# Token tiles in blocks of 1, eight times 2, and 1, instead of nine times 2, with the expert weights split further ahead in the short blocks

## The reference, cut to what matters

```python
def _moe_ref(x, w_gate, w1, w2):          # first mixture: N, D, E, F = 2304, 512, 8, 1024
    P = ...                               # gates of each token and expert, 8 rounds of normalising
    for e in range(E):
        h = np.maximum(x @ w1[e], 0.0)
        out += P[:, e:e + 1] * (h @ w2[e])
    return out

def _moe2_ref(x, phi, w1, w2):            # second mixture: 32 slots
    logits = x @ phi
    d = softmax of logits over the tokens
    slot_input = (d.T @ x).reshape(E, S_per_e, D)
    for e in range(E):
        slot_out[e] = np.maximum(slot_input[e] @ w1[e], 0.0) @ w2[e]
    c = softmax of logits over the slots
    return c @ slot_out
```

## Time and profile before

| | us |
|---|---|
| median of three runs | 1754.67 (1753.51 to 1755.44) |
| the profiled execution | 1753.28 |
| its span, first to last instruction | 1751.5 |
| PE busy | 1700.8 (97%) |
| PE weight loads (beside PE) | 1305.2 |
| DVE busy | 1024.3 (58%) |
| ACT busy | 776.9 (44%) |
| POOL busy | 418.8 (24%) |
| granted clock of PE, mean | 0.988 |
| moved by DMA | 258.57 MB |

### The profile page before, as it was taken

One profiled execution on the slowest core, in us unless ns is written; L12 is line 12 of the kernel. 1 busy time (PEld: TensorE's weight loads), 2 busy tenths in 40 slices (PEclk: granted clock), 3 DMA queues, 4 the chain that ended last, 5 costly groups with the idle time before them and its releaser, 6 DMA issues.

```text
span 1751.5 us, 31771 instructions
## 1 busy us (share of the span) xinstructions
PE 1700.8 (97%) x13225; PEld 1305.2 (75%) x13225; DVE 1024.3 (58%) x1306; ACT 776.9 (44%) x1161; POOL 418.8 (24%) x319
## 2 busy tenths in 40 slices
PE   7999999999999999999999999999999999999975
PEld 6888888888876877777777777777777777777434
DVE  6888787878754555555555555555555555555201
ACT  3444444444466444444444444454444444444101
POOL 3788888888810000000000000000000000000000
PEclk9999999999999999999999999999999999999997
DMA  9531322322035444443443444444434434454998
GB/s 300 144 82 42 79 45 65 59 46 52 15 133 193 157 151 141 142 144 133 145 145 132 155 135 141 137 141 136 145 133 146 147 131 153 156 192 167 386 420 337
DMA packets 159390, 258.57 MB, mean 148 GB/s; under 512 B 46784, under 2 KB 65216, under 8 KB 153536
## 3 DMA queue, kind: packets, MB, share of 16 engines
q1 hardware_dynamic: 159248, 256.54, 44.7%
HBM read 251.79 MB, written 9.96 MB: 149 GB/s over the span
## 4 chain that ended last, share of the span: by engine, by line
PE 63%; DMA 3%; DVE 2%; ACT 2%; issue 1%; SPq 0%; DVEq 0%
PE ring L1062 44%; PE ring L1072 7%; PE ring L1084 4%; PE ring L1119 4%; DMA wring<-in_moe_w_dram 2%; DMA xraw<-in_moe_w_dram 1%; PE ring L974 1%; DVE w_lo L1350 1%; PE ring L985 1%; ACT w_hi L1248 1%; PE ring L1170 1%; PE ring L1190 1%; ACT x_split L1240 0%; PE ring L1095 0%; ACT hring L1255 0%
## 5 line engine op out<-in xcount | busy, mean ns | idle before, releaser
L1062 PE MATMUL ring<-w_hi,x_split 128*128 128x512 f32 x2304 | 790.8, 404 | 3.3 <-DVE w_lo L1350 2.5
L1062 PEld LDWEIGHTS ring<-w_hi,x_split 128*128 128x128 f32 x2304 | 432.8, 188 | 116.7 <-issue 24.6
L1062 PE MATMUL ring<-w_lo,x_split 128*128 128x512 f32 x1152 | 449.9, 391 | 0.0
L1350 DVE TENSOR_TENSOR w_lo<-w_raw,w_hi 128x1024 fp32r<-128x1024 f32 x288 | 356.6, 1239 | 155.5 <-ACT w_hi L1248 155.5
L1293 ACT ACTIVATE wring<-ring,pw 128x512 f32<-128x512 f32 x218 | 150.1, 689 | 435.5 <-PE ring L1062 435.5
L1392 DVE COPY h_t<-ring 128x512 f32<-128x512 f32 x288 | 199.1, 691 | 236.6 <-PE ring L1072 236.5
L584 POOL TENSOR_TENSOR acc<-acc,pt 128x576 f32<-128x576 f32 x210 | 297.5, 1417 | 28.1
L1248 ACT ACTIVATE w_hi<-w_raw 128x1024 fp32r<-128x1024 f32 x288 | 302.6, 1051 | 0.0
L1528 POOL TENSOR_TENSOR x_split<-xraw,x_split 128x512 fp32r<-128x512 f32 (+1 forms) x20 | 23.6, 1185 | 980.0 <-ACT x_split L1240 980.0
L515 DVE TENSOR_REDUCE neg_part<-ring 116x2 f32<-116x768 f32 (+1 forms) x240 | 228.8, 958 | 43.7 <-PE ring L303 24.4
L1062 PEld LDWEIGHTS ring<-w_lo,x_split 128*128 128x128 f32 x1152 | 217.5, 189 | 37.9
(11 more groups left out here) (212 smaller groups left out, 1692.8 us busy)
## 6 DMA issues: line engine op xcount, KB each, us to landing
w_raw<-in_moe_w_dram SPq DMA_DIRECT2D x288, 512.0 KB, 3.5
wring<-in_moe_w_dram SPq DMA_DIRECT2D x34, 1024.0 KB, 10.0
q_raw<-in_q_dram SPq DMA_DIRECT2D x32, 288.0 KB, 5.9
v_raw<-in_v_dram SPq DMA_DIRECT2D x16, 576.0 KB, 4.5
xraw<-in_moe_w_dram SPq DMA_DIRECT2D x9, 1024.0 KB, 14.7
k_raw<-in_k_dram SPq DMA_DIRECT2D x30, 288.0 KB, 7.1
hring<-in_moe_w_dram SPq DMA_DIRECT2D x6, 1024.0 KB, 21.1
out_dram<-wring SPq DMA_DIRECT2D x8, 512.0 KB, 6.1
```

What stands on the lines that cost most here:

```text
L1062: last = pe.matmul(h_ps[n % 3][:, :], a[:, k, toks], w[:, k, :], start=(k == 0 and m == 0), stop=(k == DK - 1 and m == 2))
L1350: dve.tensor_tensor(w1_lo[v % 2][:, 2 * c:2 * c + 2, :], w1_raw[:, 2 * (p % RAWS):2 * (p % RAWS) + 2, :], w1_hi[v % 2][:, 2 * c:2 * c + 2, ...
```

## The change

The blocks become 1, eight times 2, and 1 tile: 10 blocks instead of 9, so the first mixture's weights are read ten times. In a block of one tile a unit lasts one tile; there both of its pieces are split two units ahead, four pieces ahead of the first tile, and PE waits for them one at a time. The raw ring has 4 places, the ring of hidden tiles 36 slots instead of 38. `G_AT` becomes 4, 9, 17, 25 and for a block of one 4, 9, 11, 13. With a last block of 16 tiles, five ring places are read for the last time ahead of it, and both halves of the raw ring are places. x's two buffers go by the tile's parity instead of its place in the block; in a block's last unit ACT splits x and the weights ahead of its copy. The last group of transposes of w2 @ phi moves behind the first hidden tile, the one before it to the end of its loop.

```diff
-SPARE_UNITS = [6, 7, 8, 9, 10]
+SPARE_UNITS = [10, 11, 12, 13, 14]
-    BLOCKS = [2] * (TT // 2)
+    BLOCKS = [1] + [2] * (TT // 2 - 1) + [1]
-    RAWS = 3
+    RAWS = 4
-    SLOTS_H = 38
+    SLOTS_H = 36
-    G_AT = [5, 9, 17, 25]
+    G_AT = {1: [4, 9, 11, 13], 2: [4, 9, 17, 25]}
+    SPLIT_EARLY = 4
...
+    def last_of(t):
+
+        b = max(b for b in range(NB) if T0[b] <= t)
+        return N0[b] + BLOCKS[b] * (UNITS - 1) + t - T0[b]
+
+    def single(v):
+
+        return BLOCKS[v // UNITS] == 1
+
+    def pieces_up_to(n):
+
+        b, u, i = place_of(n)
+        v = global_unit(b, u)
+        if single(v) or (i == 1 and v + 1 < UNITS * NB and single(v + 1)):
+            ahead = PIECES * (v + 3)
+        else:
+            ahead = PIECES * (v + 2) + i
+        return min(ahead, PIECES * UNITS * NB)
+
+    def pieces_at(n):
+        before = max([SPLIT_EARLY] + [pieces_up_to(m) for m in range(max(0, n - 3), n)])
+        return range(before, max(before, pieces_up_to(n)))
...
         PLACES = [("x", behind_c(i), TT) for i in range(3)] \
             + [("slots", four(i), last_user(i)) for i in EARLY_RING] \
-            + [("slots and logits", (wring[:, 22:24, :], unit_rows(4)), last_user(22, 2))] \
-            + [("raw", w1_raw[:, 0:4, :], W1_PIECES - 1)] \
+            + [("raw", w1_raw[:, 4 * i:4 * i + 4, :], W1_PIECES - 2 + 2 * i) for i in range(2)] \
...
-            EARLY_AT = [PIECES * UNITS * (NB - 1) + n for n in (6, 10, 14)]
+            EARLY_AT = [PIECES * UNITS * (NB - 1) + n for n in (4, 10, 16)]
...
-                if i % 16 == 8 and i > 16:
+                if i % 16 == 8 and 16 < i < STEPS - 16 + 8:
                     turn_phi(i // 16 - 1)
+            turn_phi(QUADS - 2)
             times_phi(QUADS - 1, (0, 1, 2, 3))
-            turn_phi(QUADS - 1)
...
                 if i == 0:
-                    pe.wait_ge(w_low, PIECES * (v + 1))
+                    pe.wait_ge(w_low, PIECES * v + 1 if single(v) else PIECES * (v + 1))
...
                 for k in range(DK):
+                    if single(v) and k == DK // PIECES:
+                        pe.wait_ge(w_low, PIECES * (v + 1))
...
                 hidden(n)
+                if n == 0:
+                    turn_phi(QUADS - 1)
...
-                if i in (18, 22, 34):
-                    split_w1((18, 22, 34).index(i))
+                if i in (18, 22, 34, 50):
+                    split_w1((18, 22, 34, 50).index(i))
...
+                urgent = u == UNITS - 1 and i == 0 and BLOCKS[b] == 2
+                if urgent:
+                    split_x(T0[b] + 2)
+                    for p in pieces_at(n):
+                        split_w1(p)
                 keep(n)
-                if u == UNITS - 1 and b + 1 < NB:
-                    split_x(b + 1, i)
+                if u == UNITS - 1 and not urgent and T0[b] + i + 2 < TT:
+                    split_x(T0[b] + i + 2)
...
-                if i == 0 and v + 1 < UNITS * NB:
-                    split_w1(PIECES * (v + 1) + 1)
-                if i == BLOCKS[b] - 1 and v + 2 < UNITS * NB:
-                    split_w1(PIECES * (v + 2))
+                for p in pieces_at(n) if not urgent else ():
+                    split_w1(p)
```

More of the change, by code:

```diff
@@ L668, in quad_before, with tokens_at @@
         return QUADS * b + u // COLS + 1
+    def last_of(t):
[14 more added lines that the diff above has]
+        return range(before, max(before, pieces_up_to(n)))
+    def tokens_at(t):
+        return slice(t % 2 * P, (t % 2 + 1) * P)
     ctx = ExitStack()
@@ L815, in last_user @@
             return max(QUADS * place_of(n)[0] + place_of(n)[1] // COLS + 1 for n in tiles)
-        RING_PLACES = sorted([i for i in range(0, 4 * (SLOTS_H // 4), 4) if i != 20], key=last_user)
+        RING_PLACES = sorted([i for i in range(0, 4 * (SLOTS_H // 4), 4) ], key=last_user)
         EARLY_RING = [i for i in RING_PLACES if last_user(i) <= G_ALL - QUADS]
         LATE_RING = [i for i in RING_PLACES if last_user(i) > G_ALL - QUADS]
-        g_rows = [wring[:, 20, :], wring[:, 21, :], w1_raw[:, 4, :], w1_raw[:, 5, :]]
+        G_PLACE = LATE_RING.pop()
+        g_rows = [four(G_PLACE)[:, q, :] for q in range(QUADS)]
         W1_PIECES = PIECES * UNITS * NB
@@ L862, in tail @@
             i = place_of_load[k]
[L863 removed]
+            return PLACES[i][1], tail_in[i], 16 * load_count[k]
         def first_load(e, n):
@@ L942, in load_tail @@
                     sp.dma_start(place_halves(place)[1], rows[:, FB // 2:FB, :]).then_inc(last_in, 16)
-                elif isinstance(place, tuple):
-                    for half, part in enumerate(place):
-                        sp.dma_start(part, rows[:, 2 * half:2 * half + 2, :]).then_inc(arrived, 16)
                 else:
@@ L1234, in _, with split_x @@
         def _(act):
[L1235 to L1240, removed]
+            def split_x(t):
+                if t >= 2:
+                    act.wait_ge(h_made, last_of(t - 2) + 1)
+                for batch, s, rows, o in tokens_of(t * P, P):
+                    last = act.activation(x_hi[:, :, tokens_at(t)][:, :, o:o + rows], xraw[:, batch * DK:(batch + 1) * DK, s:s + rows], ACT.Copy)
                 last.then_inc(x_high, 1)
@@ L1270, in _ @@
                 if i == EARLY_QUADS:
-                    for x in range(BLOCKS[0]):
-                        split_x(0, x)
-                if i in (18, 22, 34):
-                    split_w1((18, 22, 34).index(i))
+                    for x in range(2):
+                        split_x(x)
+                if i in (18, 22, 34, 50):
+                    split_w1((18, 22, 34, 50).index(i))
                 if i == 15:
@@ L1279, in _ @@
                     keep_wp(i // 16 - 1)
-                if i % 16 == 8 and i > 16:
+                if i % 16 == 8 and 16 < i < DK * UNITS - 16 + 8:
                     keep_phi(i // 16 - 1)
+            keep_phi(QUADS - 2)
             keep_wp(QUADS - 1)
@@ L1382, in _ @@
                 dve.tensor_tensor(pw[:, :, :], pw[:, :, :], col[:, :].unsqueeze(1).broadcast_to([P, TT, E]), ALU.mult).then_inc(scaled, 1)
-            for p in range(PIECES + 1):
+            for p in range(SPLIT_EARLY):
                 split_w1(p)
@@ L1473, in _ @@
                         keep_c(b - 1)
[L1474 to L1479, removed]
+                    if at in G_AT[BLOCKS[b]]:
+                        add_g(b - 1, G_AT[BLOCKS[b]].index(at), g_ps)
+                for p in pieces_at(n):
+                    split_w1(p)
             keep_turned(TILES - 1)
@@ L1522, in _ @@
             pool.memset(ones[:, :], 1.0).then_inc(ones_set, 1)
[L1523 to L1529, removed]
+            for t in range(TT):
+                pool.wait_ge(x_high, t + 1)
+                for batch, s, rows, o in tokens_of(t * P, P):
+                    at = slice(t % 2 * P + o, t % 2 * P + o + rows)
+                    last = pool.tensor_tensor(x_lo[:, :, at], xraw[:, batch * DK:(batch + 1) * DK, s:s + rows], x_hi[:, :, at].bitcast(F32), ALU.subtract)
+                last.then_inc(x_low, 1)
             pool.wait_ge(z_made, QUADS * NB)
```

24 lines of the change are left out of this document (10 added, 14 removed).

## The result

The changed kernel takes **1769.5 us** (median of six runs, 1766.9 to 1771.0) against 1755.1 before, a ratio of 1.0078 with a 95% interval from 1.0059 to 1.0098: slower by 14.5 us, where 5.9 had been forecast. The sign was right, the size was not, and the time lies outside the range of 1753 to 1768. The profiled execution took 1768.52 with a span of 1766.7, 15.2 more than before.

What follows compares the result with a forecast made beforehand. PE bounds the kernel up to the last expert tile, then the remaining weights' transfer. PE's +6.0 and waits of +1.5 put the last hidden product at 1636.3; weights end +5.9 later, giving 1760.6 us, range 1753 to 1768.

Steps and rivals of the forecast that it cites:

- The bounds and the sign: Whole kernel: PE bounds up to the last expert tile, then the remaining weights' transfer; slower by 5.9 us.
- rival 2: Tail: last piece still goes out 16.6 us ahead, so the gain pays for PE; 1756.0 us, not slower; 25%.
- the units of one tile: One-tile blocks: pieces land in 3.5 us, a raw place has 0.6 left; waits cost +1.5 for both blocks.
- Rival 1: One-tile blocks starve: a piece takes 5.8 us, waits 10 in all instead of 1.5; +14.4, 1769 us; 15%.
- partly covered: Last block: three early loads each push a piece back 2.3 us, partly hidden by some 17 us of products and logits.
- PE's work for the tenth block: PE up to the last hidden tile: products +3.7, parts of the logits +1.0, rest of a block +2.5.
- The border: Rest of the extra block (logits, both turns, waits between blocks): between half and all of 3.4 us, taken as +2.5.
- Blocks of two: Two-tile blocks: the 36-slot ring and splitting x ahead of ACT's keep cost nothing; 0.2 to 0.5 each if late.
- The start: Before the first hidden tile: moved transposes fill PE's waits for ACT; -1.2 us, at worst -0.7.
- The tail: After the last hidden tile: 48.2 MB at 418 GB/s take 115.4 us from the last piece; weights end at 1739.7.
- 7.5 us are lost: Tail of the kernel before: 121.6 us against 114.1 at 418 GB/s; added places on SP's list can win the difference.
- 415 GB/s or more in every window: Sign for the tail: from the last piece on, that rate throughout, without the earlier dip to 307 GB/s.

Runs made afterwards that it cites:

- half_pieces: Changed kernel, but in one-tile blocks only the left half of each w1 piece's columns is transferred, all instructions kept (output not the reference's); 1759.6 us.
- nine_twos: Changed kernel with its blocks put back to nine of two tiles, early loads and place list fitted to that; 1751.8 us, ratio 0.9987 to the kernel before.
- before_start: Kernel before the change plus only the moved transposes of w2 @ phi and ACT's copies; 1753.7 us against 1754.1, ratio 0.9996.
- late_third_g: Changed kernel with its third early load 6 pieces later and one-tile blocks' products at tiles 4, 7, 9, 11; 1767.3 us.

## Why the prediction was wrong

**The bounds and the sign** were right: PE up to the last hidden tile, the transfers behind it, and each us of PE's delay reaches the end. The last piece went out 12.06 us ahead of the last hidden product's end (1629.63; forecast 12.0), and rival 2, a lead of 16.6, is out.

**The step that failed is the one of the units of one tile.** It took "the landing takes 3.5" from a stretch at 140 GB/s and left a margin of 0.6 us on it. The landing is 4.9 us in the median and 6.1 at most at the double rate, so the margin is gone. Instead of +1.5 the waiting cost 6.1 (tiles of after less those of half_pieces, 1082.4 - 1076.3): 2.6 in the first block (66.5 us to its copy of z, against 63.9 in half_pieces; the same code takes 65.6 to 67.1 in the other executions) and 3.5 in the last. Rival 1's own sum gives the first block's share if the measured landing is put in: 4.9 + 1.05 + 1.22 = 7.2 us for a place per two tiles instead of 6.4, eight times 0.8, less the 3.6 of parts, some 2.5. The working had both prices at hand: the bound of rival 1 (a piece at 5.8 us) and the 2.3 us by which each early load pushes a piece back. The second was called "partly covered" by the 17 us of other work in the block; but the cover stands at certain tiles, the third load fell between them, and it pushed its piece back by 8.7 - 4.9 = 3.8 us and not by 2.3. Rival 1 is what happened, at 6.1 of the 10 us it had been given; its signs came too (landings above 4.5, and PE's idle time up by 5.2, between the 1.5 of the forecast and the 8 of the rival). It had a chance of 15%; the range cut it. That its time of 1769 nearly met the 1769.5 is luck: what its waits had too much, the tail below made up. The rule quoted from the Trainium skill, "DMA: Bandwidth & Descriptors", section "Latency and other measured facts", that HBM's latency rises at high load, pointed to 5.3 us a piece and some 5 us more in the sum. The trace shows 4.9, and 4.6 us more. Whether it is that latency or the pieces' sharing of the engines no run here separates.

**PE's work for the tenth block**: +9.0 (half_pieces' 7.0, with the 2.0 that eight blocks of two save) instead of +7.2. Two of its terms were read from one start to the next inside a run of such work, 1.75 for parts and 1.83 for a product. In the tiles' pace of half_pieces a tile with a quad of parts of 128 columns takes 4.39 instead of 3.21, which is 1.18 and not 0.89, and one with a product of a two-tile block 5.27, 2.06 and not 1.83: some 0.25 us go each time such work stands alone in a tile, which may be the price of changing from one kind of matmul to the other; no run tries that by itself. The border, taken at 2.5, was too dear: behind the one-tile block of half_pieces the two tiles with logits and the first turn take 3.66 and 3.60 us, 0.9 over two plain ones. Summed over all tiles by what stands behind their transposes, half_pieces has 6.4 us more than nine_twos in parts, products and turns of c (forecast 4.7), 1.2 more in logits and turns of d (forecast 2.5), and 1.3 more in tiles with nothing of the kind, which are waits. So the work was missed by about 0.4 only, by two errors that cancel, and the waits are rather 6.1 + 1.3 = 7.4.

**Blocks of two** were costed at nothing and are 0.25 us shorter each, -2.0 in all. The split of x ahead of ACT's copy was named for what it delays, not for what it frees. **The start**: -1.2 forecast; the first hidden tile starts 0.2 earlier in the profile, and before_start shows nothing above its uncertainty.

**The tail** was to take 103.4 us from the last hidden product and takes 107.5. Bytes and rate were right: from 1629.6 to 1748 the windows above hold 7.0 x 332 + 107.4 x 421 + 4 x 196, 48.3 MB, and 421 GB/s would carry them in 114.7 us. The stretch took 119.5. 1.5 of the 4.8 are the slow first 7 us. The other 3.3 lie between the end of the transfers, about 1745.9, and the last wait at 1749.18. Here the step of "7.5 us are lost" was at fault: 2.3 of those 7.5 stand at the end (from about 1731.5 to 1733.8 in before), and no place on a list can win them. After has one more there. PE's granted clock does not explain it: it is 0.50 (1.2 GHz) in the window from 1744 and the products there take 1.9 us instead of 1.1, but before has it at 0.50 from 1721 to 1730 and half_pieces from 1729 to 1742, and half_pieces has the shortest end of all. The time from the last hidden product to the end lies between 122.8 and 126.8 us for the other kernels with the change and the three early loads, so a term of this kind is not good to better than some 2 us, and the cause of the one us is open. Of the signs named ahead, 415 GB/s or more in every window did not come: the first 7 us have 332.

Together: +4.6 for the waits, +1.8 for PE's work and the waits that are left in half_pieces, -2.0 for the blocks of two, +1.0 for the start, +4.1 for the tail, whose last 3.3 us are partly unexplained: 9.5, against the 9.3 between the forecast for the profiled execution (1759.2) and its 1768.5.

## What to carry to other kernels

Halving the work between two transfers doubles the rate at which they are asked for; take the landing for such a chain from a stretch at that rate, and if there is none, put its range up to the nearest loaded transfer into the forecast, not a margin of 0.6 us on the unloaded one. The pace of a ring is its bytes divided by landing plus use: compute it, and hold it against what the engines move with packets of that size, before the blocks are made smaller. One more place was not tried here. And a load slipped in among urgent ones must stand ahead of tiles that have other work, tile by tile; the sum over the block says nothing.

## What was not expected of the hardware

The time from issue to landing of a 512 KB piece is 3.5 us with about one open at a time and 4.9 (up to 6.1) with 2.7 open, though the engines then move only 262 GB/s at a share of 0.78. Half a piece takes 2.9 us at the median in the one-tile block (2.5 at the least), and a load of 1 MB among the pieces 5.8. The size of the packets counts as well: with the 2 KB packets of the pieces full engines would move about 336 GB/s by the estimate above, with the 8 KB packets of the tail they move 421. And a queue of five open loads did not give the full rate at once: late_third_g ran at 330 GB/s over 4 us with them.
